# Attention with a shared score bank: all score products at the head of a step, and the second part of the row maximum kept in PSUM

## What is computed

```python
q_pool = q.reshape(B, H, S // 2, 2, D).mean(axis=3)          # B=2, H=8, S=1152, D=64
scores = 1/sqrt(D) * q_pool @ k.T                              # 576 x 1152 for each b, h
attn   = exp(scores - scores.max(-1)); attn /= attn.sum(-1) + 1e-9
x      = attn @ v                                              # 1152 tokens x 512
# then: top-1 mixture of 8 experts (relu MLP, 512 -> 1024 -> 512), gates
# then: a dense MLP 512 -> 2048 -> 512 with h * tanh(softplus(h))
```

## Time and profile before

| | |
|---|---|
| median of three executions | 700.98 us (699.46 to 701.44) |
| the profiled execution | 695.75 us |
| span from its first to its last instruction | 693.9 us |
| mean granted TensorE clock, share of 2.4 GHz | 0.997 |
| busy in the span: TensorE, VectorE, ScalarE, GpSimd | 97%, 73%, 59%, 12% |

### The profile page before, as it was taken

One profiled execution on the slowest core, in us unless ns is written; L12 is line 12 of the kernel. 1 busy time (PEld: TensorE's weight loads), 2 busy tenths in 40 slices (PEclk: granted clock), 3 DMA queues, 4 the chain that ended last, 5 costly groups with the idle time before them and its releaser, 6 DMA issues.

```text
span 693.9 us, 14849 instructions
## 1 busy us (share of the span) xinstructions
PE 674.6 (97%) x5210; PEld 596.8 (86%) x5210; DVE 506.5 (73%) x1188; ACT 409.6 (59%) x824; POOL 80.5 (12%) x115
## 2 busy tenths in 40 slices
PE   6999999999999999999999999999999999999996
PEld 5888888888888888799999898989899988899995
DVE  5667777767686776676665667586899988787874
ACT  5656575656665757646565666575666655455542
POOL 3403131304040300040000000000000000101001
PEclk9999999999999999999999999999999999999999
DMA  8677979797979420049992653031300000001001
GB/s 192 150 229 201 273 215 257 178 255 180 244 177 242 107 66 1 2 179 389 397 396 81 244 180 123 15 137 35 117 1 1 0 1 1 15 32 46 0 1 45
DMA packets 91095, 93.83 MB, mean 135 GB/s; under 512 B 41248, under 2 KB 65824, under 8 KB 90528
## 3 DMA queue, kind: packets, MB, share of 16 engines
q1 hardware_dynamic: 87280, 84.39, 41.6%
q10 hardware_dynamic: 2320, 4.00, 1.9%
q0 software_dynamic: 1440, 4.72, 1.8%
HBM read 59.80 MB, written 16.78 MB: 110 GB/s over the span
## 4 chain that ended last, share of the span: by engine, by line
PE 91%; DVE 5%; issue 1%; ACT 1%; DMA 1%; POOL 0%; DVEq 0%; SPq 0%; ACTq 0%
PE score_banks L1074 13%; PE score_banks L1044 12%; PE turn L816 12%; PE pvT L797 11%; PE score_banks L1059 10%; PE score_banks L773 5%; PE score_banks L1096 5%; PE score_banks L774 5%; PE pvT L1096 5%; PE turn L1096 4%; PE turn L737 1%; PE turn L1022 1%; PE turn L1031 1%; DMA raw_k<-k 1%; PE score_banks L971 1%
## 5 line engine op out<-in xcount | busy, mean ns | idle before, releaser
L816 PE MATMUL turn<-ident,prob 128*128 128x128 f32 x648 | 110.2, 280 | 4.3 <-DVE x_tok L1420 2.4
L1360 DVE TENSOR_REDUCE nmax_part<-score_banks 128x1 f32<-128x768 f32 x72 | 68.9, 957 | 58.9 <-PE score_banks L774 45.3
L816 PEld LDWEIGHTS turn<-ident,prob 128*128 128x128 f32 x648 | 76.4, 140 | 26.0 <-issue 13.6
L1044 PEld LDWEIGHTS score_banks<-xsT,w_slot 128*128 128x128 f32 x832 | 95.0, 192 | 3.1 <-DVE hT_lo L1604 2.0
L1044 PE MATMUL score_banks<-xsT,w_slot 128*128 x832 | 95.6, 275 | 1.6 <-DVE hT_lo L1604 1.6
L1144 ACT ACTIVATE prob<-score_banks,nmax 128x1152 f32<-128x1152 f32 x72 | 87.6, 1216 | 1.8 <-DVE nmax L1370 1.8
L797 PE MATMUL pvT<-probT,v_sb 128*64 128x128 f32 (+1 forms) x1404 | 85.9, 269 | 0.0
L1151 ACT ACTIVATE probT<-turn 128x384 f32<-128x384 f32 x72 | 35.4, 492 | 85.5 <-PE turn L816 85.3
L773 PE MATMUL score_banks<-kT,qT 128*128 128x384 f32 x192 | 79.9, 416 | 3.3 <-ACT prob L1144 2.4
L797 PEld LDWEIGHTS pvT<-probT,v_sb 128*64 128x64 f32 x1404 | 69.5, 137 | 11.9 <-issue 11.9
L1599 DVE TENSOR_TENSOR w_lo<-w_slot,w_hi 128x512 fp32r<-128x512 f32 x104 | 69.2, 688 | 3.1 <-ACT w_hi L1268 3.0
(11 more groups left out here) (241 smaller groups left out, 1380.6 us busy)
## 6 DMA issues: line engine op xcount, KB each, us to landing
w_slot<-moe_w SPq DMA_DIRECT2D x16, 2048.0 KB, 16.6
slots_dram<-zeros SPq DMA_DIRECT2D x8, 1472.0 KB, 11.3
raw_k<-k SPq DMA_DIRECT2D x16, 288.0 KB, 5.9
v_sb<-v SPq DMA_DIRECT2D x16, 288.0 KB, 4.1
w_in_sb<-moe_w_in SPq DMA_DIRECT2D x2, 2048.0 KB, 8.0
w_out_sb<-moe_w_out SPq DMA_DIRECT2D x2, 2048.0 KB, 9.5
kT<-k_hi SPq DMA_DIRECT2D x14, 288.0 KB, 4.2
kT<-k_lo SPq DMA_DIRECT2D x14, 288.0 KB, 5.1
```

The source lines that it names most:

```text
L816: last = pe.transpose(bank[:, j * P:(j + 1) * P], prob[:, s % 2, c * KC + j * P:c * KC + (j + 1) * P], ident[:, :])
L1044: last = pe.matmul(h1_bank[f % 4][:, 0:P], w1_e[:, d, f * P:(f + 1) * P], xsT[:, d, bass.ds((t % XS_RING) * P, P)], start=(d == 0), stop=( ...
L1360: dve.tensor_reduce(nmax_part[:, s, 0:1], scores[s % 2][:, lo:lo + 2, 0:KC], AX.XY, ALU.max, negate=True).then_inc(max_part, 1)
```

## The change

In one step of TensorE the three score chunks now stand together at the head, ahead of all transpositions: `qk(s + 1, 2)`, `qk(s + 2, 0)`, `qk(s + 2, 1)`. ScalarE makes `exp(s + 1)` at the head of its step, ahead of both copies of transposed probabilities. In the last iteration the turn of the last columns of x (`turn_last_d(0)`) and its copy (`copy_last_d(0)`) move from the end of step 15 to the head of step 16, the copy behind the exponential. VectorE's program keeps its order; `max_rest` writes its result into column 384 of the score bank that it has read (512 columns wide, 384 used), and the minimum is a `tensor_scalar` that reads that column from PSUM and the first part as a scalar from SBUF. `nmax_part` has one number per tile.

```diff
@@ TensorE, pe_body
                     pe.wait_ge(exp_done, g + 1)
-                    if first and s == 0:
-                        pe.wait_ge(first_ready, FIRST_TURN0_FREE)
-                    else:
-                        pe.wait_ge(pt_copied_act, 2 * g)
-                    last = turn_p(s, 0)
-                    if out_of:
-                        last = turn_o(out_of[0], it - out_of[1], turn[0])
-                    last.then_inc(p_turned, 1)
+                    if not (final and s == SB - 1):
+                        qk((s + 1) % SB, 2)
                     if next_tile:
...
                         if not (first and s == 0):
                             qk((s + 2) % SB, 0)
-
+                            qk((s + 2) % SB, 1)
+                    if final and s == SB - 2:
+                        pe.wait_ge(x_written, NIT * GB - 3)
+                        turn_last_d(0)
+
+                    if first and s == 0:
+                        pe.wait_ge(first_ready, FIRST_TURN0_FREE)
+                    else:
+                        pe.wait_ge(pt_copied_act, 2 * g)
+                    last = turn_p(s, 0)
+                    if out_of:
+                        last = turn_o(out_of[0], it - out_of[1], turn[0])
+                    last.then_inc(p_turned, 1)
...
-                    if next_tile:
-                        if first and s == 0:
-                            pe.wait_ge(first_ready, FIRST_PAIR_READY)
-                            qk(2, 0)
-                        qk((s + 2) % SB, 1)
+                    if first and s == 0:
+                        pe.wait_ge(first_ready, FIRST_PAIR_READY)
+                        qk(2, 0)
+                        qk(2, 1)
...
-                    if next_tile:
-                        pe.wait_ge(exp_done, g + 2)
-                        qk((s + 2) % SB, 2)
-                    if final and s == SB - 3:
-                        pe.wait_ge(x_written, NIT * GB - 3)
-                        turn_last_d(0)
@@ TensorE, ahead of the first step
-            pe.wait_ge(exp_done, 1)
-            qk(1, 2)
@@ ScalarE, act_body
                     g = SB * it + s
+                    if not (final and s == SB - 1):
+                        exp((s + 1) % SB, g + 1)
+                    if final and s == SB - 2:
+                        copy_last_d(0)
                     act.wait_ge(p_turned, NC * g + 2)
                     act.activation(probT[:, pt_of[s], KC:2 * KC], turn[1][:, 0:KC], ACT.Copy).then_inc(pt_copied_act, 1)
-                    if not (final and s == SB - 1):
-                        exp((s + 1) % SB, g + 1)
...
-                    if final and s == SB - 3:
-                        copy_last_d(0)
@@ VectorE, max_first and max_rest
-                dve.tensor_reduce(nmax_part[:, s, 0:1], scores[s % 2][:, lo:lo + 2, 0:KC], AX.XY, ALU.max,
+                dve.tensor_reduce(nmax_part[:, s:s + 1], scores[s % 2][:, lo:lo + 2, 0:KC], AX.XY, ALU.max,
...
-                dve.tensor_reduce(nmax_part[:, s, 1:2], scores[s % 2][:, c, 0:KC], AX.X, ALU.max,
+                dve.tensor_reduce(scores[s % 2][:, c, KC:KC + 1], scores[s % 2][:, c, 0:KC], AX.X, ALU.max,
...
-                dve.tensor_tensor(nmax[:, s:s + 1], nmax_part[:, s, 0:1], nmax_part[:, s, 1:2], ALU.min
+                dve.tensor_scalar(nmax[:, s:s + 1], scores[s % 2][:, c, KC:KC + 1], nmax_part[:, s:s + 1], None, ALU.min
```

More of the change, by code:

```diff
@@ L99, in build @@
         nmax = sb("nmax", [P, SB], F32)
-        nmax_part = sb("nmax_part", [P, SB, 2], F32)
+        nmax_part = sb("nmax_part", [P, SB], F32)
         rsum = sb("rsum", [P, SB], F32)
```

## The result

| | before | changed |
|---|---|---|
| median beside each other (12 executions each) | 701.14 us | 698.38 us (695.1 to 700.25) |
| ratio, 95% interval | | 0.9958 (0.9941 to 0.9976) |
| the profiled execution, its span | 695.75, 693.9 us | 699.61, 697.8 us |

The change makes the kernel faster by 0.42%, 2.9 us. The profiled execution of the changed kernel is slower than that of the kernel before, against the medians, so the stages are read apart. The milestones are rows of three lines: the exponential (its fourth start and its last enclose the attention proper) and the first and last product of the MLP. First the kernel before: instructions of each line, duration in ns, min/median/max, first and last start in us.

The account below looks back on a forecast made before the run. TensorE's own work was taken as the bound, busy 262.7 of 266.0 us. Removable waits of 3.3 to 7.1 us, middle 5.2, less 0.3 (L1401) and 0.5 (the end), gave -4.4: 696.6 us from 700.98, range 693.6 to 700.6.

Parts of the forecast that it names:

- the shared bank's wait: Ahead of each TensorE step, `qk(s + 1, 2)` keeps its place and its wait for the exponential; only two more pairs follow.
- The gain in the attention: TensorE's removable waits in the attention: 3.3 us of idle products at least, 7.1 us at most, middle 5.2.
- over 7 us could come only from cheaper changes of kind: Sign against the prediction: the attention shortening by more than 7 us, which only cheaper product-transposition changes can give.
- The minimum: On VectorE, reading one number from PSUM: the 1.5 us minima held by GpSimd go; each costs an estimated 0.06 us more.
- The chain in a step: From first score product through maximum, minimum and exponential to TensorE's next use: 2.80 us, against steps of 3.35 or 3.68.
- its cover: ScalarE's copy of chunk 1 releases the preparation at 3.20 us, TensorE arrives at 3.35: 0.15 us spare, cost taken as 0.
- The rival in which ScalarE's copy stops TensorE: Copy of chunk 1 holds the 44 preparation steps if its chain exceeds 3.35 us; up to 705 us; chance 0.10.
- The changes of kind: On TensorE, 116 fewer switches between transpositions and products, at most 0.01 us each; bounds 0 and 1.2 us, taken as 0.
- The rival: Changes of kind on TensorE do cost, 0.08 us each: 9.3 us more would go, to 687 us; chance 0.07.
- The end: In step 16 ScalarE's copy of x's last columns delays a waiting preparation: 0.5 us, between 0 and 1.
- Start-up: Before the attention proper, both versions wait for the second exponential at the same place: 0.
- From there on nothing changes: After the attention, which ends some 4 us earlier, the rest of the kernel keeps its times.

Follow-up runs that it names:

- a_split: The changed kernel with GpSimd's split of a head put ahead of its q sum for the next head: 693.82 us, ratio to the kernel before 0.9906.
- a_lateload: The changed kernel, GpSimd untouched, with the 4 MB load of the first expert's weights issued later: ratio to the kernel before 0.9929.
- a_again: The changed kernel itself, unchanged, run once more on another chip: ratio to the kernel before 0.9966.
- a_twomin: The changed kernel with GpSimd's split first and each minimum made twice, once into an unused tile: ratio to the kernel before 0.9917.
- a_mid: The changed kernel with GpSimd's split first, but score pairs `qk(s + 2, 1)` back behind the third turned chunk: ratio to the kernel before 0.9979.
- a_split2: The changed kernel with GpSimd's split first, measured a second time: 688.39 us, ratio to the kernel before 0.9908.
- min_only: The kernel before with only the new minimum, which reads one operand from PSUM: ratio to the kernel before 0.9959.
- order_only: The changed kernel with the old minimum, both operands in SBUF: 702.08 us, ratio to the kernel before 1.002.

## Why the prediction came out as it did

The size was about right (-4.4 us forecast, -2.9 measured), but by luck, as a sum of two errors. The attention was to give all of it, and gave 1.3 us of which the start took 1.0; the MLP was to give nothing, and gave 2.1.

**The step that failed** is the sentence on the shared bank's wait, with which the part on TensorE's order ends: "No work of TensorE is queued differently behind it except that two more pairs now follow it." Those pairs are where the next head begins, and in that step they wait for the next head's k and q to be in place. That wait is not among the rows of the kernel before, because there the transfer was over half a us early; its slack was never priced. The changed kernel comes 1.7 us sooner and its transfer 2.7 us later. a_split and a_lateload show the cost from two sides. The price was 6.0 us (257.0 to 250.9): 3.8 of standing still, and by an estimate 1.5 for the 3.1 us of halved clock behind it; the rest is not traced. a_again shows the same with more of both: 4.6 us of standing still, then this window, and an attention of 258.7 us, 7.8 more than a_split's.

```profile
83.20:88.80 5.60, 5.60 (x32) 4.84 (x33) 1.10 (x5) 0.49 (x1) 0.00 (x0) 0.50 0.91 294
```

**The gain in the attention** was put at 3.3 to 7.1 us. With the transfer out of the way it is 258.3 - 250.9 = 7.4, a little over the upper bound. That fits if all of the loads' waits were real time, and the issue gaps' 0.03 us too; it was inferred from the sum, not measured part by part. The prediction also said that over 7 us could come only from cheaper changes of kind. a_split passes 7 us without them, so that sign was drawn too sharply.

**The minimum** was read rightly. Its maximum is 222 ns in 72, none is held by GpSimd, and `write_x` had been the right neighbour. The Trainium skill ("VectorE: DVE Perf Modes", section on the TRN2 errata) gives a VectorE instruction a fixed cost of 120 cycles with a source in PSUM and 58 with one in SBUF. By an estimate from it that is 0.06 us more, and the trace agrees: 219 against 159 ns.

**The chain in a step** was right to some hundredths of a us, its cover was not. A step of the changed kernel that begins a group, from the first product of `qk(s + 1, 2)`:

```profile
103.57 0.42 PE L773 MATMUL score_banks<-kT,qT 128*128 128x384 f32 x1
...
104.20 0.57 DVE L1364 TENSOR_REDUCE score_banks<-score_banks 128x1 f32<-128x384 f32 x1
...
104.80 0.22 DVE L1367 TENSOR_SCALAR nmax<-score_banks,nmax_part 128x1 f32<-128x1 f32 x1
...
105.05 1.22 ACT L1141 ACTIVATE prob<-score_banks,nmax 128x1152 f32<-128x1152 f32 x1 [0.66 <-DVE nmax L1367]
...
106.26 0.48 ACT L1152 ACTIVATE probT<-turn 128x384 f32<-128x384 f32 x1
...
106.85 0.36 PEld L737 LDWEIGHTS turn<-ident,raw_k 128*128 128x128 f32 x3
106.96 0.49 PE L737 MATMUL turn<-ident,raw_k 128*128 128x128 f32 x3
...
107.20 0.42 PE L773 MATMUL score_banks<-kT,qT 128*128 128x384 f32 x1
```

The exponential starts 1.48 us behind the first product (1.44 forecast, 1.50 with the longer minimum), the copy of chunk 1 ends at 3.17 (3.20 less the 0.05 for the load), the preparation starts at 3.39 (3.35), the step takes 3.63 (3.68). But the prediction set the moment at which the load may start (3.20) against the start of the preparation's product (3.35), and the load starts ahead of its product, here by 0.11 us. The cover is 106.85 - 106.74 - 0.05 = 0.06 us where 0.15 was said. It was enough for the changed kernel (0.6 us of listed waits in the whole attention), so the term of 0 in the sum stands. The rival in which ScalarE's copy stops TensorE had its place right and was nearer than it was put: a_twomin's chain, 0.13 us longer, already reaches it.

**The changes of kind** were rightly put at nothing; the starts in a_mid agree. The rival had this much to it that the place of a pair is worth 6 us, but by VectorE's waiting.

**The end** was put at 0.5 us: the turn of x's columns (L896) waits 0.5. **L1401** (now L1398) at 0.3: no wait of TensorE goes back to it. **Start-up** at 0: +1.0 in these two traces, but the fourth exponential starts anywhere from 24.5 to 27.7 us in the four traces of the changed order with the new minimum and both pairs at the head (changed, a_again, a_split, a_split2), so nothing can be said.

**"From there on nothing changes"** was wrong. All nine traces with the new minimum have an MLP of 201.15 to 201.45 us, all five with the old one 203.51 to 203.59. It is not a wait; the products themselves follow each other closer. Before, then the changed kernel, then a_twomin, the same products of the MLP's second half:

```profile
L1096 PE MATMUL score_banks<-w_out_lo,g_hi x48: 389/397/397, 494.9 to 685.1; 128*128 128x512 f32 x48
L1096 PE MATMUL score_banks<-w_out_hi,g_lo x48: 389/397/397, 495.2 to 685.4; 128*128 128x512 f32 x48
```

```profile
L1093 PE MATMUL score_banks<-w_out_lo,g_hi x48: 389/395/395, 500.9 to 689.0; 128*128 128x512 f32 x48
L1093 PE MATMUL score_banks<-w_out_hi,g_lo x48: 389/393/397, 501.1 to 689.2; 128*128 128x512 f32 x48
```

```profile
L1094 PE MATMUL score_banks<-w_out_lo,g_hi x48: 388/389/394, 492.7 to 680.5; 128*128 128x512 f32 x48
L1094 PE MATMUL score_banks<-w_out_hi,g_lo x48: 388/389/397, 492.9 to 680.7; 128*128 128x512 f32 x48
```

A few ns in each of some 1000 products (576 and 432) are the 2.1 us. The MLP's instructions and their shapes are the same in all. What differs there is where tiles lie in SBUF: `nmax_part` has one number per tile for two, its place shrinks from 160 to 96 bytes per partition, and every tile behind it, the MLP's weights and `g_hi`, `g_lo` among them, lies 64 bytes lower; a_twomin's extra tile moves them up by 96, and its products have a third pattern. min_only and order_only tie the gain to the minimum's edit and not to the order. That the addresses are the cause is an argument from these three placements. No kernel was run in which padding alone is changed, so it stays open.

**What else stays open.** a_split2's trace is 7.3 + 2.1 + 0.7 us (attention, MLP, start) = 10.1 us shorter than before's outside the third stage, and the medians beside each other differ by 6.4. The profiled execution of a_split2 is 1.6 us under its median, that of the kernel before 0.9 us over the 694.84 of that set, and its third stage is 1.1 us shorter; these make up the difference. What varies between executions of one kernel is open; the number of minima that meet GpSimd, and the stretches of halved clock, are candidates.

## What to carry to other kernels

An engine that is made to arrive earlier meets waits that no view of the old profile lists, because there they were just over. Ahead of such a change, go through the semaphores that the moved work passes and read for each when its producer was done and when it was asked for; slack of half a us is a bound. When the expected gain does not come, look for one long wait before many small ones: here one in a single head ate 6 of 7 us, and the cure lay in the order of an engine that is busy 12% of the time. And read a gain stage by stage: the total agreed with the forecast while its stages did not.

## What was not expected of the hardware

- The granted clock fell to 0.50 when TensorE had stood still for 3.75 us, though it had been busy without a gap from 70 us on; the wait costs about 6 us, not 4. In a_again, after 4.6 us, it stayed at 0.50 until 88.9 us.
- The MLP's products of 512 columns take 227 or 231 ns from start to start (medians) in kernels that differ there by the addresses of tiles alone, as far as is known; the stage differs by 1%.
- Two minima behind one another on VectorE, of 0.22 us each, start 0.13 us apart, so the second adds 0.13 us to a chain.
- A two-operand instruction of VectorE with both numbers in SBUF, one per partition, took up to 1.54 us beside GpSimd (1.50 in order_only); the form with one operand in PSUM never took over 223 ns in the nine traces that have it.
